# Another order of TensorE's, ScalarE's and VectorE's pieces within a head's turn of the attention

## The reference, cut to what matters

```python
q_assign = argmax(q_n . c_n); k_assign = argmax(k_n . c_n)      # 16 centroids a head
mask = q_assign[:, None] == k_assign[None, :]
scores = where(mask, q @ k.T / sqrt(64), -1e9)
attn = exp(scores - max(scores)); attn = attn / sum(attn)
out = attn @ v
x = moe(out rows by token); return moe2(x)      # logits of the gate are x @ w_gate
```

## Time and profile before

| | |
|---|---|
| median of 3 runs | 1081.56 us (1081.26 to 1088.33) |
| the profiled execution | 1083.52 us, its span 1081.7 us |
| attention (first to last `tr_out`'s result) | up to about 321 us of the span |
| TensorE, matmuls / weight loads | 94% / 86% of the span |

### The profile page before, as it was taken

The page is one execution under the profiler, slowest core; times in us unless marked ns, Lnnn a source line. Parts: engine busy times, 40 slices in busy tenths (PEclk is TensorE's granted clock), DMA queues, the critical chain, the costliest instruction groups (busy, mean ns, idle before and its releaser), DMA issues.

```text
span 1081.7 us, 17912 instructions
## 1 busy us (share of the span) xinstructions
PE 1017.8 (94%) x6410; PEld 932.3 (86%) x6410; DVE 620.5 (57%) x1302; ACT 490.7 (45%) x963; POOL 442.0 (41%) x363
## 2 busy tenths in 40 slices
PE   3899999999987998999999999999999999999996
PEld 3888888888876897999899988899999888999995
DVE  3778788878877443555214444555559445555542
ACT  3787887888752331333643232233324332333220
POOL 7031313132200011111266685666556756665542
PEclk9999999999996798999999999999999999999998
DMA  3323232222135632445962212221222222212201
GB/s 98 81 74 82 73 80 73 73 76 77 36 75 167 204 110 77 171 171 171 270 150 78 78 40 78 79 71 61 65 78 78 98 79 78 68 62 66 78 1 59
DMA packets 87745, 99.61 MB, mean 92 GB/s; under 512 B 18560, under 2 KB 57472, under 8 KB 87680
## 3 DMA queue, kind: packets, MB, share of 16 engines
q1 hardware_dynamic: 84976, 92.40, 28.9%
q0 software_dynamic: 2704, 6.33, 1.9%
HBM read 79.81 MB, written 6.32 MB: 80 GB/s over the span
## 4 chain that ended last, share of the span: by engine, by line
PE 80%; ACT 11%; issue 3%; DVE 2%; DMA 2%; POOL 1%; ACTq 0%; SPq 0%; DVEq 0%
PE ps_y L1397 9%; PE ps_y L1396 9%; PE ps_y L1395 9%; PE ps_h L1422 8%; PE ps_y L1437 6%; PE ps_h L1397 6%; PE ps_h L1395 6%; PE ps_h L1396 6%; PE ps_t L1310 4%; ACT probs L691 3%; PE ps_s L1297 3%; ACT p_hi L704 2%; PE ps_m L1344 2%; PE ps_m L1271 2%; PE ps_o L1324 2%
## 5 line engine op out<-in xcount | busy, mean ns | idle before, releaser
L557 POOL TENSOR_TENSOR w_lo<-w_sum,w_hi 128x1792 fp32r<-128x1792 f32 x32 | 129.8, 4079 | 62.3 <-ACT w_hi L764 62.3
L1397 PE MATMUL ps_y<-b_lo,h_hi 128*128 128x512 f32 x384 | 149.7, 390 | 0.0
L1396 PE MATMUL ps_y<-b_hi,h_lo 128*128 128x512 f32 x384 | 149.7, 390 | 0.0
L1395 PE MATMUL ps_y<-b_hi,h_hi 128*128 128x512 f32 x384 | 149.4, 389 | 0.0
L1221 DVE SCALAR_TENSOR_TENSOR Y<-ps_y,mix_n,Y 128x512 f32<-128x512 f32 x84 | 63.0, 750 | 134.9 <-PE ps_y L1397 134.9
L1395 PE MATMUL ps_h<-x_hi,w_hi 128*128 128x384 f32 x384 | 128.6, 335 | 0.0
L1397 PE MATMUL ps_h<-x_lo,w_hi 128*128 128x384 f32 x384 | 128.5, 335 | 0.0
L1396 PE MATMUL ps_h<-x_hi,w_lo 128*128 128x384 f32 x384 | 128.4, 334 | 0.0
L969 DVE TENSOR_TENSOR p_lo<-ps_t,p_hi 128x384 fp32r<-128x384 f32 x192 | 101.7, 549 | 36.2 <-ACT p_hi L704 36.1
L563 POOL TENSOR_TENSOR b_lo<-b_raw,b_hi 128x2048 fp32r<-128x2048 f32 x16 | 74.0, 4626 | 115.7 <-ACT b_hi L771 114.9
L704 ACT CAST p_hi<-ps_t 128x384 fp32r<-128x384 f32 x192 | 86.4, 481 | 55.6 <-PE ps_t L1310 54.6
(11 more groups left out here) (194 smaller groups left out, 2305.3 us busy)
## 6 DMA issues: line engine op xcount, KB each, us to landing
w_sum<-in_moe_w_dram SPq DMA_DIRECT2D x64, 256.0 KB, 3.1
b_raw<-in_moe_w_dram SPq DMA_DIRECT2D x16, 1024.0 KB, 5.2
raw_a<-in_moe_w_dram SPq DMA_DIRECT2D x8, 1024.0 KB, 6.7
raw_b<-in_moe_w_dram SPq DMA_DIRECT2D x8, 1024.0 KB
odd_a<-in_moe_w_dram SPq DMA_DIRECT2D x8, 1024.0 KB, 6.5
odd_b<-in_moe_w_dram SPq DMA_DIRECT2D x8, 1024.0 KB
khhT<-kqT SPq DMA_DIRECT2D x32, 192.0 KB, 2.9
raw_k<-in_k_dram SPq DMA_DIRECT2D x16, 192.0 KB, 2.4
```

The costliest lines, as they stand in the source:

```text
L557: g.tensor_tensor(w_lo[t][:], w_sum[t][:, 1:8], w_hi[t][:].bitcast(F32), ALU.subtract).then_inc(wlo_done[t], 1)
L1395: t_.matmul(dst, w_hi, x_hi, start=first, stop=False)
L1396: t_.matmul(dst, w_lo, x_hi, start=False, stop=False)
L1397: return t_.matmul(dst, w_hi, x_lo, start=False, stop=last)
```

## The change

Only the order of calls in the three `turn` functions is changed. ScalarE's and VectorE's lists are also cut at another place: `exp_tile(soon, 5)` and `hi_half(soon, 4, 1)` from the end of a turn stand as `exp_tile(now, 5)` and `hi_half(now, 4, 1)` at the start of the next, and likewise the pieces of VectorE's list from `max_tile(later, 1)` on. What is left besides that cut:

- TensorE: `tr_probs(now, 5, 1)` before `tr_probs(soon, 0, 0)`; `tr_probs(soon, 0, 1)` before `tr_out(now, 0)`; `scores(soon, 3)` before `tr_probs(soon, 1, 0)`; `tr_probs(soon, 1, 1)` before `scores(soon, 4)`; both halves of `tr_probs(soon, 2)` before `values(now, 1, 0)`; `values(soon, 0, 0)` before `tr_probs(soon, 3, 1)`.
- ScalarE: `hi_half(now, 5, 1)` before `hi_half(soon, 0, 0)`; `copy_far_k(later)` before `hi_half(soon, 3, 1)`.
- VectorE: `lo_half(now, 5, 1)` before `lo_half(soon, 0, 0)`; `lo_half(soon, 1, 1)` before `max_tile(soon, 4)`; `lo_half(soon, 3, 0)` before `max_tile(soon, 5)`; `row_scale` and `lo_half(soon, 4, 1)` before `lo_half(soon, 5, 0)`.

```diff
--- before.py
+++ after.py
@@ -714,12 +714,14 @@
 
             def turn(h, b):
                 now, soon, later = (near(h, b, d) for d in range(3))
+                exp_tile(now, 5)
+                hi_half(now, 4, 1)
                 hi_half(now, 5, 0)
                 exp_tile(soon, 0)
                 copy_tr(later, 0)
                 take_oT(now, 0)
+                hi_half(now, 5, 1)
                 hi_half(soon, 0, 0)
-                hi_half(now, 5, 1)
                 copy_tr(later, 1)
                 exp_tile(soon, 1)
                 hi_half(soon, 0, 1)
@@ -734,11 +736,9 @@
                 take_oT(now, 1)
                 copy_own_q(later)
                 hi_half(soon, 3, 0)
+                copy_far_k(later)
                 hi_half(soon, 3, 1)
-                copy_far_k(later)
                 hi_half(soon, 4, 0)
-                exp_tile(soon, 5)
-                hi_half(soon, 4, 1)
 
             for n in range(-2, 2):
                 turn(n // 2, n % 2)
@@ -992,29 +992,29 @@
 
             def turn(h, b):
                 now, soon, later = (near(h, b, d) for d in range(3))
+                max_tile(soon, 1)
+                lo_half(now, 5, 1)
+                lo_half(soon, 0, 0)
+                max_tile(soon, 2)
+                rows_out(now, 0)
+                lo_half(soon, 0, 1)
+                max_tile(soon, 3)
+                lo_half(soon, 1, 0)
+                lo_half(soon, 1, 1)
                 max_tile(soon, 4)
-                lo_half(soon, 1, 1)
                 cluster_sums(later)
                 own_cluster(later)
                 lo_half(soon, 2, 0)
                 lo_half(soon, 2, 1)
+                lo_half(soon, 3, 0)
                 max_tile(soon, 5)
-                lo_half(soon, 3, 0)
                 lo_half(soon, 3, 1)
                 lo_half(soon, 4, 0)
                 max_tile(later, 0)
                 rows_out(now, 1)
-                lo_half(soon, 5, 0)
                 row_scale(soon)
                 lo_half(soon, 4, 1)
-                max_tile(later, 1)
-                lo_half(later, 0, 0)
-                lo_half(soon, 5, 1)
-                max_tile(later, 2)
-                rows_out(soon, 0)
-                lo_half(later, 0, 1)
-                max_tile(later, 3)
-                lo_half(later, 1, 0)
+                lo_half(soon, 5, 0)
 
             for n in range(-2, 2):
                 turn(n // 2, n % 2)
@@ -1352,27 +1352,27 @@
                 values(now, 0, 1)
                 tr_rows(later, 0)
                 scores(soon, 1)
+                tr_probs(now, 5, 1)
                 tr_probs(soon, 0, 0)
-                tr_probs(now, 5, 1)
                 tr_rows(later, 1)
                 scores(soon, 2)
+                tr_probs(soon, 0, 1)
                 tr_out(now, 0)
-                tr_probs(soon, 0, 1)
+                scores(soon, 3)
                 tr_probs(soon, 1, 0)
-                scores(soon, 3)
                 tr_rows(later, 2)
+                tr_probs(soon, 1, 1)
                 scores(soon, 4)
-                tr_probs(soon, 1, 1)
                 clusters(later)
-                values(now, 1, 0)
                 tr_probs(soon, 2, 0)
                 tr_probs(soon, 2, 1)
+                values(now, 1, 0)
                 values(now, 1, 1)
                 tr_own(later)
                 scores(soon, 5)
                 tr_probs(soon, 3, 0)
+                values(soon, 0, 0)
                 tr_probs(soon, 3, 1)
-                values(soon, 0, 0)
                 tr_probs(soon, 4, 0)
                 scores(later, 0)
 
```

## The result

The changed kernel took 1067.61 us (median of 4 runs, 1064.32 to 1069.68) against 1081.41 us (4 runs, 1079.54 to 1088.33). The ratio is 0.9848, 95% interval 0.9813 to 0.9883: 1.2 to 1.9% less time. The forecast was 1066.5 us, range 1062 to 1076. The profiled execution had a span of 1064.9 us, 16.8 less than before.

What follows compares the result with a forecast made beforehand. TensorE's stream, with stalls seen in its weight loads, was taken as the bound. A turn of 17.30 instead of 18.33 us saves 14.4 over 14 turns, plus 0.6 at the ends: 15.0 off 1081.56 gives 1066.5 us, range 1062 to 1076.

Steps and rivals of the forecast that it cites:

- late starts: TensorE's weight loads starting after the previous block's stream ends: 2.29 us a turn without the branch, the most to gain.
- First half: `scores(later, 0)` to `clusters`: 9.46 us forecast against 10.03 before without the branch, a gain of 0.57 us.
- the sum: Block lengths and engine distances laid through one attention turn: 17.04 us, or 17.15 with half the 0.23 us branch.
- a tie: Exp of tile 1 ready before `scores(soon, 3)` within 0.1 us, so no stall was put there.
- Second half: `clusters` to the next `scores(later, 0)`, reached at 17.04 us; stalls of 0.43 before `tr_own`, 0.13 before `tr_probs(soon, 4, 0)`.
- the allowance for the ties: 0.15 us a turn for four near-simultaneous arrivals and ScalarE's and VectorE's loop branches, making the turn 17.30 us.
- its sign: Loads of `clusters` in the attention should come every 17.2 to 17.4 us.
- late next: VectorE's row in the second half: `tr_own` at 13.89 us, TensorE stalling 0.43 us there instead of 0.16.
- VectorE's row as the bound: Rival, chance 0.20: VectorE from tile 1's maximum to `tr_own` loses at every handover; 17.9 us a turn, 1075.5 us.
- Not additive: Rival, chance 0.08: halves don't add, or the `take_oT` and `copy_own_q` chain ends unchanged; 18.2 to 18.3 us a turn.
- Slower through the maximum of tile 5: Rival, chance 0.05: VectorE's maximum behind `lo_half(soon, 3, 0)` delays exp of tile 5; 0.45 us more a turn, 1088 us.
- called free: Second half, TensorE's swap of `values(soon, 0, 0)` and `tr_probs(soon, 3, 1)` costs nothing, its `hi_half` standing behind `copy_far_k`.

Runs made afterwards that it cites:

- further swap: Changed kernel with `tr_rows(later, 2)` ahead of `tr_probs(soon, 1, 0)` on TensorE and `copy_tr(later, 2)` ahead of `hi_half(soon, 1, 0)` on ScalarE: turn 17.09 us, median 1066.14 us.
- the second half alone: Changed kernel with the old order put back from `scores(later, 0)` to `clusters` on all three engines: turn 17.65 us against 18.33 before, span 1080.4 us.
- the kernel whose TensorE stalls 1.45 us a turn: Changed kernel with ScalarE's `copy_far_k(later)` put back behind `hi_half(soon, 3, 1)`: mean turn 18.49 us, span 1088.6 us.

## Why the prediction was right

**The bound.** TensorE's stream with its late starts, read from the weight loads, was the right account: what the changed orders took away were late starts. How much room there was is less well shown. The loads promised up to 2.29 us a turn, the matmul column 1.1; the forecast of 1.03 was below both, and the change took 1.18, hardly more than the matmul column allowed. What speaks for the loads is what is left: in the turn from 118.67 to 135.77 the matmul column is idle for 0.08 us, while 17.10 - 15.92 = 1.18 us lie outside the weight loads, and the further swap still took 0.05 out of the turn. The rule of the Trainium skill (page "Perfetto Trace Analysis", section "Identifying the Most-Contended Engine") agrees with this, by that small margin; no run shows how much of the rest can be had.

**First half.** From `scores(later, 0)` to `clusters` the sum gave 9.46. Measured: 135.77 - 126.26 = 9.51 without the branch, and 118.67 - 109.02 = 9.65 with it (0.14 there, 109.80 against 109.02 + 0.64). The sum was better than its parts, and that is luck. `tr_probs(soon, 0, 1)` stalls 0.12, not 0.25, since `lo_half` to load is 0.60 here and not 0.67. `scores(soon, 3)`, called a tie, waits 0.18 to 0.26 us for exp of tile 1. The stall of 0.05 to 0.15 before `clusters` wasn't in the sum. And the third `tr_rows` was given 0.49 us (7.97 to 8.46), the length of its loads in the row, where its stream takes 0.36 (117.24 to 117.60). The errors of 0.13 and 0.13 on one side cancel those on the other.

**Second half.** From `clusters` to the next scores the sum gave 17.04 - 9.46 = 7.58; measured 126.26 - 118.67 = 7.59 and, one turn on, 143.38 - 135.77 = 7.61. Without the branch `tr_own` comes at 140.09 - 126.26 = 13.83, forecast 13.89, and exp of tile 5 at 17.68, forecast 17.6 (17.79 with the branch). Here the parts fit too, but for the stalls: 0.20 to 0.28 before `tr_own` instead of 0.4, and as much before `tr_probs(soon, 4, 0)` instead of 0.1.

**What was wrong.** First, the allowance for the ties: 0.15 us a turn were added to 17.15, and the turn is 17.14, below the 17.2 to 17.4 that the prediction named as its sign. Without the branch the turn is 143.38 - 126.26 = 17.12 against a sum of 17.04, so ties and small waits cost 0.08, and the branch costs 0.14 every second turn instead of 0.23. That makes the gain in the attention too small: 15.0 us forecast, 16.6 measured from turn 0 to the last `tr_out`. The measured median gain was 13.8, from times that scatter by 5 us; so the forecast lies between, and the closeness of 1066.5 to 1067.6 owes something to that. Second, the sentence that VectorE's row is "late next". Its time was right and its role was not: `tr_own`'s loads start at 122.89 and its three transposes last 0.34 us, so `copy_own_q` could begin before 123.3; it begins at 123.55, behind `take_oT`, which waits for `values`. The further swap, where `tr_own` waits longer and the turn gets shorter, agrees. Third, moving the maximum of tile 5 was priced as a risk and was neither risk nor gain. Fourth, a reading: the stall before `scores(soon, 4)` was taken from the bracket, 0.27. By the prediction's own lengths (122.02 + 0.37 for `tr_rows`) the start was 0.39 late.

**The rivals.** VectorE's row as the bound: it asked for 17.9 us a turn with the second half's gain lost; the turn is 17.14 and the second half alone gives 0.67. Not additive: it asked for 18.2 or more, and 0.67 + 0.52 stand against 1.18. Slower through the maximum of tile 5: refuted, 17.15 without it and 17.14 with it. A slower kernel was near in another place, which the prediction called free: `values(soon, 0, 0)` ahead of `tr_probs(soon, 3, 1)` costs 0.86 us a turn unless ScalarE does `copy_far_k` first; the prediction gave the reason for its cost of nothing, not the price without it.

## What to carry to other kernels

Where several engines run fixed lists, price a new order by laying it on measured distances between engines (producer's start to consumer's start, from the trace of before) and follow the late chain by hand; here that gave each half of the turn within 0.05 us, in the first half with parts that were off by up to 0.26 and cancelled. A swap on one engine can harm while another engine keeps its old order (0.86 us here), so undo such swaps both singly and together. Measure a repeated stage by its period in one profile and not by the run's time: it repeated to 0.01 us here, where the time scatters by 5. Look at the single periods and their granted clock too: one slow turn in thirteen moved a mean by 0.13 us.

## What the runs showed that was not expected

The branch of the loop cost TensorE 0.23 us before and 0.14 in the changed kernel. In the kernel with the third `tr_rows` first, the part from 108.36 to 109.14 still shows it, but turns with and without the branch differ by under 0.1 us (17.12 and 17.08): the waits behind it seem to cover it. The granted clock 100 to 120 us behind the attention was 0.74 and 0.91 in two executions of one program. And inside the attention it fell once, to 0.50 for about 2 us, in the kernel whose TensorE stalls 1.45 us a turn, in one of its thirteen turns.
